# Experts' stage of a fused attention and mixture-of-experts kernel: the items walked expert by expert with nested branches, PSUM banks assigned anew, and a ring of ten pieces for the weights

## What is computed

```python
N, D, E, F = (1536, 512, 8, 1024)
cap = N // E * 2                     # 384 rows per expert
...
expert_idx = np.argmax(logits, axis=1)
...
for i in range(N):
    e = expert_idx[i]
    if counts[e] < capacity:
        disp[e, counts[e]] = x[i]
...
h = np.maximum(np.einsum('ecd,edf->ecf', disp, w1), 0.0)
y = np.einsum('ecf,efd->ecd', h, w2)
...
        out[i] = gate_w[i] * y[expert_idx[i], pos[i]]
```

## Time and profile before

| | us |
|---|---|
| time, median of 3 runs | 657.99 (657.54 to 659.1) |
| the profiled execution, its time | 657.53 |
| its span | 655.8 |
| first `expert_in` matmul starts | 437.98 |
| last `expert_out` matmul ends | 645.13 |
| PE busy over the span | 603.6 (92%) |

### The profile page before, as it was taken

One profiled execution on the slowest core, in us unless ns is written; L12 is line 12 of the kernel. 1 busy time (PEld: TensorE's weight loads), 2 busy tenths in 40 slices (PEclk: granted clock), 3 DMA queues, 4 the chain that ended last, 5 costly groups with the idle time before them and its releaser, 6 DMA issues.

```text
span 655.8 us, 11641 instructions
## 1 busy us (share of the span) xinstructions
PE 603.6 (92%) x3901; PEld 509.3 (78%) x3901; DVE 353.9 (54%) x1035; ACT 283.8 (43%) x681; POOL 140.2 (21%) x188
## 2 busy tenths in 40 slices
PE   8779899999999999999999999989999879859983
PEld 6568788888888888888888999878777667647762
DVE  4668676565556555655564464436726455473410
ACT  5655455433433343434332211417836464465420
POOL 4332222212112222222221000031112231230012
PEclk9989899999999999999999999899999889879998
DMA  6534340201052311011000400246846756765100
GB/s 178 147 81 129 114 130 17 65 17 36 18 160 65 81 52 31 17 33 50 1 17 1 161 0 1 82 161 189 294 161 219 264 173 211 260 205 197 40 33 18
DMA packets 73393, 67.37 MB, mean 103 GB/s; under 512 B 43012, under 2 KB 49172, under 8 KB 73328
## 3 DMA queue, kind: packets, MB, share of 16 engines
q1 hardware_dynamic: 69488, 57.76, 28.4%
q0 software_dynamic: 3840, 8.77, 4.7%
HBM read 57.75 MB, written 12.58 MB: 107 GB/s over the span
## 4 chain that ended last, share of the span: by engine, by line
PE 82%; issue 6%; ACT 4%; DVE 4%; DMA 2%; POOL 1%; ACTq 0%; SPq 0%; DVEq 0%; POOLq 0%
PE bank L858 21%; PE bank L860 20%; PE bank L859 20%; PE bank L848 9%; PE bank L926 4%; PE bank L898 3%; PE bank L992 2%; ACT wh L653 1%; DVE wl L1152 1%; DMA fw<-y_scratch,mask 1%; DMA fw<-in_moe_w_in_dram 1%; DVE rw L1173 1%; PE bank L941 1%; ACT rw L662 0%; ACT fw L686 0%
## 5 line engine op out<-in xcount | busy, mean ns | idle before, releaser
L858 PE MATMUL bank<-wh,rw 128*128 128x512 f32 x416 | 170.2, 409 | 11.3 <-issue 6.2
L860 PE MATMUL bank<-wh,rw 128*128 128x512 f32 x416 | 165.6, 398 | 0.0
L859 PE MATMUL bank<-wl,rw 128*128 128x512 f32 x416 | 165.5, 398 | 0.0
L1152 DVE TENSOR_TENSOR wl<-fw,wh 128x512 fp32r<-128x512 f32 x160 | 100.5, 687 | 49.8 <-ACT wh L653 47.3
L858 PE MATMUL bank<-rw,wh 128*128 128x256 f32 x384 | 113.0, 294 | 0.3 <-DVE rw L1228 0.3
L860 PE MATMUL bank<-rw,wl 128*128 128x256 f32 x384 | 108.6, 283 | 0.0
L859 PE MATMUL bank<-rw,wh 128*128 128x256 f32 x384 | 108.4, 282 | 0.0
L858 PEld LDWEIGHTS bank<-wh,rw 128*128 128x128 f32 x416 | 80.1, 192 | 29.2 <-issue 13.2
L768 ACT CAST rw<-fw 128x256 fp32r<-128x256 f32 x96 | 39.0, 406 | 145.4 <-DVE fw L1346 145.1
L860 PEld LDWEIGHTS bank<-wh,rw 128*128 128x128 f32 x416 | 79.7, 192 | 18.0
L562 POOL TENSOR_SCALAR fw<-fw,rinv 128x256 f32<-128x256 f32 (+1 forms) x88 | 77.1, 887 | 71.8 <-DVE rinv L1207 71.7
(11 more groups left out here) (114 smaller groups left out, 630.6 us busy)
## 6 DMA issues: line engine op xcount, KB each, us to landing
fw<-in_moe_w_dram SPq DMA_DIRECT2D x128, 256.0 KB
fw<-in_moe_w_in_dram SPq DMA_DIRECT2D x16, 256.0 KB, 3.0
fw<-in_moe_w_out_dram SPq DMA_DIRECT2D x16, 256.0 KB, 2.7
o_sb<-in_q_dram SPq DMA_DIRECT2D x12, 256.0 KB, 3.2
o_sb<-in_k_dram SPq DMA_DIRECT2D x12, 256.0 KB, 3.8
y_scratch<-fw SPq DMA_DIRECT2D x12, 256.0 KB, 2.1
out_dram<-v_or_route SPq DMA_DIRECT2D x12, 256.0 KB, 3.4
v_raw<-in_v_dram SPq DMA_DIRECT2D x11, 256.0 KB, 3.0
```

The source lines that it names most:

```text
L858: pe.matmul(dst, ah, bh, start=start, stop=False, skip_group_check=True)
L859: pe.matmul(dst, ah, bl, start=False, stop=False, skip_group_check=True)
L860: return pe.matmul(dst, al, bh, start=False, stop=stop, skip_group_check=True)
L1152: dve.tensor_tensor(wl[:, hf, col:col + PIECE], staged, f32(wh[:, hf, col:col + PIECE]), ALU.subtract).then_inc(weights_low_split, 1)
```

## The change

The experts' stage gets another order, other buffers and other branches; what is computed stays the same, and nothing ahead of the stage moves but the number of pieces of the first expert loaded ahead (ten, not eight).

- **Order.** All engines walk expert by expert. On PE an expert's turn is: half of `expert_in` of item 0, `slot_T` of item 1 if real, the other half, `slot_T` of the next expert's item 0, `expert_out` of the previous expert's last real item (`last_of`), `hidden_T` of item 0, `slot_T` of item 2 if real, and then for j = 1, 2, if real, a body `another(j)`: `expert_in(j)`, `expert_out(j-1)`, `hidden_T(j)`. ACT's turn is written to match.
- **Branches.** `more_than` runs a body or raises the semaphores it would have raised; `last_of` is two nested branches, each with its copy of the step, and raises the semaphore of the empty items behind it.
- **Banks and buffers.** Hidden values have one pair of banks (`bk[0:2]`) and one `h_sb`; `hT` is one pair instead of two; the transposed rows have three banks and four `eT`. So `expert_in` waits for the ReLU of *every* item before it, where it waited for those up to two before.
- **Ring.** `stage2` has ten places (two of them in `v_raw`). `gather` follows `X_ORDER`.

The core of the diff:

```diff
-    STG2 = 8
+    STGF, STG2 = 8, 10
...
+        X_ORDER = [0]
+        for e in range(E):
+            X_ORDER += [TPE * e + 1] + [TPE * (e + 1)] * (e + 1 < E) + list(range(TPE * e + 2, TPE * (e + 1)))
+        X_AT = {i: k for k, i in enumerate(X_ORDER)}
+        HT_BANK, X_BANK = bk[4:6], (bk[2], bk[3], bk[6])
...
+            def more_than(self, e, j, real, *skipped):
                 with self.eng.If(self.count[e] > j * P):
-                    stage_of(i)
+                    real()
                 with self.eng.Else():
+                    self.mark(*skipped)
+
+            def last_of(self, e, finish, done):
+
+                i = TPE * e
+                with self.eng.If(self.count[e] > 2 * P):
+                    finish(i + 2)
+                with self.eng.Else():
+                    with self.eng.If(self.count[e] > P):
+                        finish(i + 1)
+                        self.mark(done)
+                    with self.eng.Else():
+                        finish(i)
+                        self.mark(done, done)
+
+            def mark(self, *skipped):
+                for done in skipped:
                     self.eng.drain().then_inc(done, 1)
...
         def _(act):
+            for e in range(E):
+                first = TPE * e
+
+                def another(j):
+                    relu(first + j)
+                    scaled(first + j - 1)
+                    hidden_high(first + j)
+
+                if e == 0:
+                    some(4, 0)
+                    busy.more_than(0, 1, lambda: x_high(1), slot_x_high_split)
+                    some(2, 0)
+                    relu(0)
+                    x_high(TPE)
+                    some(2, 0)
+                    some(2, 1)
+                else:
+                    relu(first)
+                    busy.more_than(e, 1, lambda: x_high(first + 1), slot_x_high_split)
+                    if e + 1 < E:
+                        x_high(first + TPE)
+                    some(KC * FP2, e + 1)
+                    busy.last_of(e - 1, scaled, expert_out_scaled)
+                hidden_high(first)
+                busy.more_than(e, 2, lambda: x_high(first + 2), slot_x_high_split)
+                some(NF2 if e else 2 * NF2 - 2, e + 1)
+                for j in range(1, TPE):
+                    busy.more_than(e, j, lambda: another(j), expert_relu_done, expert_hidden_high_split)
+            busy.last_of(E - 1, scaled, expert_out_scaled)
...
         def _(pe):
             def expert_in(i, halves=(0, 1)):
                 e, j = ITEMS[i]
-                pe.wait_ge(slot_x_low_split, i + 1)
-                if i >= 2:
-                    pe.wait_ge(expert_relu_done, i - 1)
+                k = X_AT[i]
+                pe.wait_ge(slot_x_low_split, k + 1)
+                if i:
+                    pe.wait_ge(expert_relu_done, i)
...
+            for e in range(E):
+                first = TPE * e
+
+                def another(j):
+                    expert_in(first + j)
+                    expert_out(first + j - 1)
+                    hidden_T(first + j)
+
+                expert_in(first, (0,))
+                busy.more_than(e, 1, lambda: slot_T(first + 1), slot_x_transposed)
+                expert_in(first, (1,))
+                if e + 1 < E:
+                    slot_T(first + TPE)
+                if e:
+                    busy.last_of(e - 1, expert_out, expert_out_done)
+                hidden_T(first)
+                busy.more_than(e, 2, lambda: slot_T(first + 2), slot_x_transposed)
+                for j in range(1, TPE):
+                    busy.more_than(e, j, lambda: another(j), expert_hidden_done, expert_hidden_transposed)
+            busy.last_of(E - 1, expert_out, expert_out_done)
```

More of the change, by code:

```diff
@@ L112, in sparse_attention_then_two_expert_layers @@
         at = 0
-        eT = [r_view(2 * D).rearrange("p (s n) -> p s n", s=2) for _ in range(2)]
-        hT = [[r_view(F2) for _ in range(2)] for _ in range(2)]
+        eT = [r_view(2 * D).rearrange("p (s n) -> p s n", s=2) for _ in range(4)]
+        hT = [r_view(F2) for _ in range(2)]
         v_raw = sb("v_raw", [P, 2, H, DH])
@@ L1120, in expert_out @@
                     col = KC * F2 + f * D
[L1121 removed]
+                    r = three(P_BANK[:, :], (hT[0][:, cs], hT[1][:, cs]),
                               (wh[:, e % 2, col:col + D], wl[:, e % 2, col:col + D]),
@@ L1404, in _ @@
             busy = Busy(dve)
-            busy.run(x_low2, 1, slot_x_low_split)
-            some(NF2 // 2, 0)
-            busy.run(x_low2, 2, slot_x_low_split)
-            some(NF2 - NF2 // 2, 0)
-            busy.run(hidden_low, 0, expert_hidden_low_split)
-            busy.run(x_low2, 3, slot_x_low_split)
-            some(KC * FP2, 1)
-            for i, (e, j) in enumerate(ITEMS):
-                if i + 1 < NA:
-                    busy.run(hidden_low, i + 1, expert_hidden_low_split)
-                if i + 4 < NA:
-                    busy.run(x_low2, i + 4, slot_x_low_split)
-                some(share(j), e + 1 + j)
+            for e in range(E):
+                first = TPE * e
+                if e == 0:
+                    some(4, 0)
+                busy.more_than(e, 1, lambda: x_low2(first + 1), slot_x_low_split)
+                if e == 0:
+                    some(2, 0)
+                if e + 1 < E:
+                    x_low2(first + TPE)
+                if e == 0:
+                    some(2, 0)
+                    some(2, 1)
+                else:
+                    some(KC * FP2, e + 1)
+                hidden_low(first)
+                busy.more_than(e, 2, lambda: x_low2(first + 2), slot_x_low_split)
+                some(NF2 if e else 2 * NF2 - 2, e + 1)
+                for j in range(1, TPE):
+                    busy.more_than(e, j, lambda: hidden_low(first + j), expert_hidden_low_split)
 def r32(ap):
```

99 lines of the change are left out of this document (40 added, 59 removed).

## The result

The changed kernel takes 665.91 us, median of 4 runs (665.52 to 668.75), the kernel before 658.55 (657.54 to 659.48): ratio 1.0121, 95% interval 1.0089 to 1.0154, so 1.2% slower, 7.4 us between the medians. The prediction was 667.5 in a range of 661 to 676.

What follows compares the result with a forecast made beforehand. PE was taken to bound the kernel. New excess (stage time beyond PE's full-rate work) summed to 43.5 us against 34.0, 9.5 more: span 665.3, profiled time 667.0, median 667.5 us, range 661 to 676.

Steps and rivals of the forecast that it cites:

- branches: Along PE's stream, 14 exposed empty steps and 16 taken branches cost 7.9 us, lower end 5.4.
- `hidden_T(0)`: In expert 0, PE waits for the ReLU one row-transpose group behind `expert_in(0)`: 0.95 us.
- `hidden_T(1)`: In expert 0, PE waits for relu(1), which stands behind 14 pieces on ACT: 0.3 to 3 us, taken as 1.5.
- behind experts 1, 3: Next `expert_in` waits for the empty third item's semaphore, raised behind `hidden_high`: 1.55 us twice, 3.1.
- behind experts 2, 4, 5: Next `expert_in` waits for empty items' semaphores that ACT raises behind eight pieces: 6.06 us three times, 18.2.
- the end: Item 21's `expert_out` directly follows its `hidden_T`, so PE waits 2.7 us ahead of it.
- clock: Low PE clock behind three long gaps, 2.5 us each, and the end's, 1.6: 9.2 us unrounded.
- expert 0: Waits ahead of `hidden_T(0)`, 0.95 us, and of relu(1) behind 14 pieces, 1.5 us with up to 3 possible.
- The ring of ten costs or gains nothing: Ten places for weight pieces: no effect, since ACT's one wait, 1.74 us, came where PE did not wait.
- the rival on DMA: DMA paces the eight pieces; three long waits grow 2.3 us each, 8.4 more with expert 0: 675.9 us; chance 0.12.
- The rival of code fetches: Seven exposed `last_of` jumps each wait 2.1 us for a fetch: 682.2 us, or 674.8 at half; chance 0.08.

Runs made afterwards that it cites:

- the filled kernel: Changed kernel with 44 transposes of the identity (12 at the last expert) in PE's arm of an empty item 1; 659.49 us, ratio 1.0032.
- the repaired kernel: Changed kernel with PE, not ACT, raising the empty items' semaphore `expert_relu_done`; 657.51 us, ratio 1.0001.
- the one with 16: Kernel with PE raising the semaphore and relu(1) early, plus 16 transposes run in PE's arm of an empty item 1; 649.61 us, ratio 0.9870.
- the padded one: Kernel with PE raising the semaphore and relu(1) early, plus 16 never-run transposes ending `another(1)` for experts 2, 4, 5, 7; 652.25 us, ratio 0.9897.

## Why the prediction was right, point by point

The mechanism and the sign were right, and the sum came within 1 us: from 437.86 to 653.17 + 0.39 are 215.7 us, less 173.1 of work 42.6 us of excess, where 43.5 were forecast; before it was 34.0. The span grew by 8.4 us, 9.5 were forecast; the rest of the 1.6 us between the forecast 667.5 and 665.91 comes from the half microsecond that was added to get from the profiled execution to the median.

| term | forecast | measured, gap + 0.16 where it is a gap |
|---|---|---|
| branches | 7.9 | 5.6 |
| `hidden_T(0)` | 0.95 | 1.4 |
| `hidden_T(1)` | 1.5 | 2.6 |
| behind experts 1, 3 | 3.1 | 2.8 |
| behind experts 2, 4, 5 | 18.2 | 18.4 |
| the end | 2.7 | 4.0 |
| clock | 9.2 | 8.2 |

The measured terms add up to 43.0 by single gaps; the clock is the difference to the filled kernel, stretch by stretch. Three were mis-sized, by 2.3 us too much for the branches and by 2.9 too little for expert 0 and the end. That these cancel is luck: the sum is nearer than its terms. **Branches:** priced from two stretches of before in which PE was idle already; `last_of`'s branches come before the work that they choose and run ahead while PE is busy, no gap stands between `slot_T` and `expert_out` of experts 4 and 6. What shows is behind drains: seven gaps of 0.37 to 0.61 us and four of 0.23, and most of it stays without any branch, as the kernel built that way shows. **Expert 0:** ACT was still at a piece when `expert_in(0)` ended, and the 14 pieces waited for DMA (0.2 to 0.6 us a time), as the upper bound of 3 allowed. **The end:** hidden rows were split after 2.4 us as forecast, but a branch of 1.9 us held PE 1.3 us longer.

*Behind experts 2, 4 and 5*, the term that made the sign, is shown by two runs: with no branch at all the gaps stay at 5.8 us, and with the semaphore raised elsewhere no gap waits for ACT. *Clock* is shown by the filled kernel, which is 6 us faster by the medians and 7.6 in the stage, where 7 to 8.5 were expected. *The ring of ten costs or gains nothing* was wrong: it gains 7 us in this order, since a long gap ends with ACT's eighth piece and with eight places that piece is late. The prediction found no use for it because ACT's one wait for a piece before did not reach PE. That the rival on DMA did not come about is owed to the ring: with eight places ACT waits 7.4 us for pieces, and two of the gaps grow by half of the 2.3 us of that rival.

*The rival of code fetches* was weighed too lightly, and on the wrong jumps: it was priced at `last_of`, with one stretch of before against it. In the changed kernel two of 62 branches of PE waited, one under ACT's gap and one at the end, 1.3 us in all in the open. It was the gain of the repaired kernel that it took: 657.5 instead of 643 to 645. The stretch of before that spoke against it could not test it: no packet of q8 runs in the 1.42 us ahead of 575.71, the next one starts at 576.83. The Trainium skill (Runtime: NRT & Kernel Launch, Instruction fetch mechanics) says that a taken branch whose target is outside the window of prefetched code waits for a DMA fetch before execution goes on; these traces agree, with 14 branches of 1.7 to 4.2 us and at each a code packet that ends 1.3 to 1.6 us before the branch does. Two things removed the long branches: PE working while the packet ran (the kernel filled with 44 transposes; the end of the one with 16), and code moved so that the packet ran earlier (the first two places of the one with 16). Each is read from the profile of one execution.

The gain of the order itself is real: without branches the old order takes 651.6 us and the new one, with the semaphore raised by PE and relu(1) early, 636.8, 2.3% less (2.5% by the ratios to the kernel before). In the kernel as changed it went into three waits of 6 us for a semaphore that stands for no work, and the low clock behind them. The best kernel here that still branches on the counts takes 649.6 us, 1.3% less than before.

The third of the one-item places never had a long branch (gaps of 1.5 us there with PE raising): its packet starts behind both branches, at 583.68 in the kernel in which PE raises. Open: which address of the code sets a packet off, since the profiles do not show where in the code a packet lies; and why a stop of 0.9 us follows the packet there in the kernel in which PE raises and not in the padded one (packet at 585.63).

## What to carry to other kernels

A semaphore that counts skipped work should be raised by the engine that would wait for it, or at the place in order where its last real predecessor is done, never behind other work; price a skipped step by what stands ahead of its mark. Look at what lies under a wait before counting its removal as gain; here a branch of 3 to 4 us lay under 6 us of ACT, and 8.4 us were gained of the 21 to 23 expected. Where code is jumped over in pieces of a hundred instructions, read the longest compare-and-branch, not the median, and look in the DMA view for the packets of kind instruction: a fetch costs where the engine has nothing else to do. Work between two such jumps can cover it, or the code can be moved; which of the two helped has to be read from the packets, not from the time.

## What the runs showed of the hardware

PE's compare-and-branch takes 0.19 us at the median, ACT's and DVE's 0.04 and 0.05, and single ones on PE take 1.7 to 4.2 us where bodies of about 100 instructions are jumped over in a row. At each of these 14 a packet of 16384 bytes runs on the instruction queue q8 (0.9 to 2.0 us), and the branch ends 1.3 to 1.6 us after it. The stage has 7 such packets in a kernel without branches, 13 in the kernel before and 16 in the changed one. With 44 transposes (5.0 us) between the jumps the packets run under them and no branch lasts over 0.44 us.

A gap of 5.97 us on PE is followed by 1.6 to 2.8 us lost at the 1.2 GHz level, measured against the same stretch of the kernel in which the gap is filled with transposes of the identity, and one of 3.82 by 1.6; filled, the gap is followed by none. Behind a gap of 2.2 to 2.5 us the loss came or did not: 1.6 us in two profiles (gaps of 2.19 and 2.46), none in the changed kernel (2.40).
